# Second MLP of an attention and two-MLP kernel: second products one product later, second high part behind p1, right sums on VectorE, left sums behind a low part

## The reference

```
def _moe2_ref(x, w_a, w_b, w_out):      # x: 2304 x 512, w_a, w_b: 512 x 1536, w_out: 1536 x 512
    a = x @ w_a
    b = x @ w_b
    return (a * b @ w_out).astype(np.float32)
```

## Time and profile before

| what | value |
|---|---|
| median of 3 runs | 998.17 us (997.8 to 999.19) |
| the profiled execution | 996.64 us, span 994.9 us |
| TensorE matmul, weight load | 962.3 us (97%), 899.5 us (90%) |
| VectorE, ScalarE, GpSimd | 609.9, 469.0, 195.4 us |
| lines 704 and 720 (matmuls of the second MLP) | 294.4 and 181.4 us |
| mean granted clock of TensorE | 0.989 of full speed |

### The profile page before, as it was taken

One profiled execution on the slowest core, in us unless ns is written; L12 is line 12 of the kernel. 1 busy time (PEld: TensorE's weight loads), 2 busy tenths in 40 slices (PEclk: granted clock), 3 DMA queues, 4 the chain that ended last, 5 costly groups with the idle time before them and its releaser, 6 DMA issues.

```text
span 994.9 us, 18268 instructions
## 1 busy us (share of the span) xinstructions
PE 962.3 (97%) x6896; PEld 899.5 (90%) x6896; DVE 609.9 (61%) x1075; ACT 469.0 (47%) x1112; POOL 195.4 (20%) x228
## 2 busy tenths in 40 slices
PE   6699999999999999999999999999999999999998
PEld 5589999999999999999999989999889998899996
DVE  5778656556656656555637676556765557656552
ACT  4667544545454545454434544344533334543432
POOL 2200211001210011200034072222262222222210
PEclk9699999999999999999999999999999999999999
DMA  8245220111300122101041132222442222322201
GB/s 197 86 142 148 67 68 19 43 48 38 91 20 22 41 73 61 44 18 50 8 152 33 56 127 64 64 72 70 131 133 74 65 64 64 127 65 64 66 30 64
DMA packets 129351, 71.40 MB, mean 72 GB/s; under 512 B 63248, under 2 KB 120304, under 8 KB 129264
## 3 DMA queue, kind: packets, MB, share of 16 engines
q1 hardware_dynamic: 128224, 69.94, 24.5%
q10 hardware_dynamic: 1040, 0.29, 0.1%
HBM read 60.76 MB, written 9.44 MB: 71 GB/s over the span
## 4 chain that ended last, share of the span: by engine, by line
PE 81%; ACT 8%; DVE 6%; issue 3%; DMA 1%; SPq 0%; POOL 0%; ACTq 0%; DVEq 0%
PE bank L704 23%; PE bank L662 18%; PE bank L648 18%; PE bank L720 14%; ACT sml L763 2%; PE bank L561 2%; PE bank L616 1%; PE bank L567 1%; PE bank L599 1%; PE bank L609 1%; ACT smp L754 1%; DVE wx L1119 1%; PE bank L541 1%; DMA out<-y 1%; DVE wx L1028 1%
## 5 line engine op out<-in xcount | busy, mean ns | idle before, releaser
L704 PE MATMUL bank<-wx 128*128 128x384 f32 x1512 | 294.4, 337 | 1.9 <-DVE c L1112 0.8
L704 PEld LDWEIGHTS bank<-wx 128*128 128x128 f32 x1512 | 268.7, 188 | 19.8 <-ACT u L931 1.6
L648 PE MATMUL bank<-wx 128*128 128x288 f32 x1536 | 231.4, 300 | 0.8 <-ACT relu L851 0.8
L662 PE MATMUL bank<-g_hi,wx 128*128 128x288 f32 x1024 | 231.9, 302 | 0.0
L648 PEld LDWEIGHTS bank<-wx 128*128 128x128 f32 x1536 | 212.3, 190 | 4.6 <-ACT relu L851 1.0
L720 PE MATMUL bank<-wx 128*128 128x512 f32 x648 | 181.4, 398 | 3.7 <-DVE wx L1119 3.1
L662 PEld LDWEIGHTS bank<-g_hi,wx 128*128 128x128 f32 x1024 | 171.4, 188 | 3.5
L1163 POOL TENSOR_TENSOR raw<-raw 128x256 f32<-128x256 f32 x144 | 111.6, 796 | 312.8 <-DMA raw<-in_moe_w_out 309.9
L662 PE MATMUL bank<-g_lo,wx 128*128 128x288 f32 x512 | 151.5, 296 | 0.0
L720 PEld LDWEIGHTS bank<-wx 128*128 128x128 f32 x648 | 116.9, 187 | 23.9 <-DVE wx L1119 10.3
L1033 DVE TENSOR_TENSOR wx<-raw,wx 128x768 fp32r<-128x768 f32 x108 | 106.7, 1014 | 40.3 <-ACT wx L833 39.6
(11 more groups left out here) (69 smaller groups left out, 923.7 us busy)
## 6 DMA issues: line engine op xcount, KB each, us to landing
raw<-in_moe_w_b SPq DMA_DIRECT2D x72, 128.0 KB, 2.2
raw<-in_moe_w_a SPq DMA_DIRECT2D x72, 128.0 KB, 2.3
raw<-in_moe_w_out SPq DMA_DIRECT2D x36, 256.0 KB, 2.8
vnat<-in_v SPq DMA_DIRECT2D x32, 144.0 KB
o_transposed<-o_sb SPq DMA_DIRECT2D x8, 576.0 KB, 3.1
o_raw<-o_transposed SPq DMA_DIRECT2D x6, 768.0 KB, 5.3
out<-y SPq DMA_DIRECT2D x18, 256.0 KB, 2.2
natq<-in_q SPq DMA_DIRECT2D x63, 72.0 KB, 2.1
```

The costliest lines, as they stand in the source:

```text
L648: mm = nc.tensor.matmul(HB[:, 0:HALF], wi(w, kd, f), xs(x, c % 2)[:, kd], start=(kd == 0 and j == 0), stop=(kd == KD - 1 and j == 2))
L662: mm = nc.tensor.matmul(ACC[o][:, 0:HALF], wo(w, f, o), g[:, slot % GB, :], start=(f == 0 and j == 0), stop=(f == F1 - 1 and j == 2))
L704: mm = nc.tensor.matmul(dst, left(w, n, a, kd), right(x, i)[:, kd * HC:(kd + 1) * HC], start=(opens and kd == 0 and m == 0), stop=(kd == K ...
```

## The change

Five edits, which belong together:

- TensorE: the second products of the step before begin behind product 1 instead of product 0; tiles 2 and 3 stand together behind product 3.
- ScalarE: the high part of `prod[1]` of a step stands behind the p1 copy of the next step, instead of behind the high part of `prod[0]`.
- VectorE: c12 stands ahead of the low part of `prod[0]` (but in the last step), and that of `prod[1]` is still last, which now waits for ScalarE's later high part.
- The right operands' sums are VectorE's: one in each of the slots 5 to 8 of the first MLP's last chunk, and one in each of steps 4 to 7 of chunks 0 and 1, ahead of c22.
- GpSimd: from block 3 on, the left sums of block n wait for the low part of `prod[0]` of step n - 3.

```diff
--- before.py
+++ after.py
@@ -728,7 +728,7 @@
                 for i in range(N7):
                     product(n, i)
                     if n > 0:
-                        for tt in ((0,), (1,), (2,), (3,), (4, 5), (), ())[i]:
+                        for tt in ((), (0,), (1,), (2, 3), (4, 5), (), ())[i]:
                             down_2(n - 1, tt)
             for tt in range(TT):
                 down_2(STEPS - 1, tt)
@@ -894,6 +894,12 @@
                 past(act, y_stored[tt % 3], 16 * (2 * c + tt // 3))
                 nc.scalar.activation(y[:, tt % 3, :], ACC2[tt], ACT.Copy).then_inc(y_ready, 1)
 
+            def split_product_hi(n, h):
+                act.wait_ge((pr1_ready, pr2_ready)[h], n + 1)
+                if n >= 2:
+                    p_free(n - 2)
+                nc.scalar.activation(p_hi[:, n % 2, h], prod[h], ACT.Copy).then_inc(ph_ready, 1)
             for n in range(STEPS):
                 c, f = divmod(n, F2)
                 renew = f == F2 - 1 and c + 1 < NC2
@@ -901,6 +907,8 @@
                 act.wait_ge(up_done, N7 * n + 1)
                 past(act, c11_ready, n)
                 nc.scalar.activation(p1_sb, X_BANK, ACT.Copy).then_inc(p1_taken, 1)
+                if n > 0:
+                    split_product_hi(n - 1, 1)
                 if renew:
                     split_right_hi(c + 1, 0)
                 if over:
@@ -931,14 +939,11 @@
                 nc.scalar.activation(u3_sb, X_BANK, ACT.Copy).then_inc(u3_taken, 1)
                 if over:
                     take_y(c - 1, 3)
-                for h, ready in enumerate((pr1_ready, pr2_ready)):
-                    act.wait_ge(ready, n + 1)
-                    if n >= 2:
-                        p_free(n - 2)
-                    nc.scalar.activation(p_hi[:, n % 2, h], prod[h], ACT.Copy).then_inc(ph_ready, 1)
+                split_product_hi(n, 0)
                 if over:
                     take_y(c - 1, 4)
                     take_y(c - 1, 5)
+            split_product_hi(STEPS - 1, 1)
             for tt in range(TT):
                 take_y(NC2 - 1, tt)
 
@@ -1032,6 +1037,13 @@
                 dve.wait_ge(w2_hi, PIECES * n + i + 1)
                 nc.vector.tensor_tensor(piece2(LO, n, i), raw[:, n % RB, LEFT + i * PIECE:LEFT + (i + 1) * PIECE],
                                         piece2(HI, n, i).bitcast(f32), ALU.subtract).then_inc(w2_lo, 1)
+            def right_sum(c, k):
+                name, a, b_ = (("t1", "b12", "b11"), ("t3", "b22", "b12"), ("t2", "b22", "t1"), ("t4", "b21", "t2"))[k]
+                dve.wait_ge(oraw_in, 32 * (c + 1))
+                if k >= 2:
+                    dve.wait_ge(t_ready, 4 * c + 2 * k - 3)
+                nc.vector.tensor_tensor(right_raw(name), right_raw(a), right_raw(b_), ALU.subtract).then_inc(t_ready, 1)
 
             def split_right_lo(c, j):
                 dve.wait_ge(x2h, N7 * c + j + 1)
@@ -1079,11 +1091,18 @@
                 attention(2 * slot + 1)
                 split_g_lo(slot)
                 if c == NCH - 1:
+                    if 5 <= f < 9:
+                        right_sum(0, f - 5)
                     for piece in early_pieces(f):
                         split_w2_lo(*divmod(piece, PIECES))
                     for j in early_rights(f):
                         split_right_lo(0, j)
             take_acc(NCH - 1)
+            def split_product_lo(n, h):
+                dve.wait_ge(ph_ready, 2 * n + 1 + h)
+                nc.vector.tensor_tensor(p_lo[:, n % 2, h], prod[h], p_hi[:, n % 2, h].bitcast(f32), ALU.subtract)\
+                  .then_inc(pl_ready, 1)
 
             for n in range(STEPS):
                 c, f = divmod(n, F2)
@@ -1108,6 +1127,8 @@
                 if n + 2 < STEPS:
                     split_w2_lo(n + 2, 0)
                     split_w2_lo(n + 2, 1)
+                if 4 <= f < 8 and c + 1 < NC2:
+                    right_sum(c + 1, f - 4)
                 dve.wait_ge(u3_taken, n + 1)
                 nc.vector.tensor_tensor(c22_sb, Y_BANK, u3_sb, ALU.add).then_inc(c22_ready, 1)
                 if renew:
@@ -1115,18 +1136,18 @@
                 dve.wait_ge(up_done, N7 * n + 6)
                 dve.wait_ge(c11_ready, n + 1)
                 nc.vector.tensor_tensor(prod[0], X_BANK, c11_sb, ALU.mult).then_inc(pr1_ready, 1)
-                dve.wait_ge(ph_ready, 2 * n + 1)
-                nc.vector.tensor_tensor(p_lo[:, n % 2, 0], prod[0], p_hi[:, n % 2, 0].bitcast(f32), ALU.subtract)\
-                  .then_inc(pl_ready, 1)
+                if n == STEPS - 1:
+                    split_product_lo(n, 0)
                 dve.wait_ge(up_done, N7 * n + 7)
                 dve.wait_ge(u2_taken, n + 1)
                 nc.vector.tensor_tensor(c12_sb, Y_BANK, u2_sb, ALU.add).then_inc(c12_ready, 1)
+                if n < STEPS - 1:
+                    split_product_lo(n, 0)
                 dve.wait_ge(c12_ready, n + 1)
                 dve.wait_ge(c22_ready, n + 1)
                 nc.vector.tensor_tensor(prod[1], c12_sb, c22_sb, ALU.mult).then_inc(pr2_ready, 1)
-                dve.wait_ge(ph_ready, 2 * n + 2)
-                nc.vector.tensor_tensor(p_lo[:, n % 2, 1], prod[1], p_hi[:, n % 2, 1].bitcast(f32), ALU.subtract)\
-                  .then_inc(pl_ready, 1)
+                split_product_lo(n, 1)
 
         @block.gpsimd
         def _(pool):
@@ -1171,28 +1192,16 @@
                 pool.wait_ge(s_ready, 4 * n + 3)
                 sum_of("s4", "a12", "s2", ALU.subtract)
 
-            def right_sums(c):
-                def sum_of(name, a, b_):
-                    nc.gpsimd.tensor_tensor(right_raw(name), right_raw(a), right_raw(b_), ALU.subtract).then_inc(t_ready, 1)
-                pool.wait_ge(oraw_in, 32 * (c + 1))
-                sum_of("t1", "b12", "b11")
-                sum_of("t3", "b22", "b12")
-                pool.wait_ge(t_ready, 4 * c + 1)
-                sum_of("t2", "b22", "t1")
-                pool.wait_ge(t_ready, 4 * c + 3)
-                sum_of("t4", "b21", "t2")
             for slot in range(SLOTS):
                 attention(2 * slot)
                 attention(2 * slot + 1)
             left_sums(0)
             left_sums(1)
-            right_sums(0)
             for n in range(2, STEPS):
+                if n >= 3:
+                    pool.wait_ge(pl_ready, 2 * (n - 3) + 1)
                 left_sums(n)
-                if n % F2 == 4 and n // F2 + 1 < NC2:
-                    right_sums(n // F2 + 1)
 
 
 # ---- launch: one core; inputs and outputs as the reference has them ----
```

## The result

The changed kernel takes 985.24 us (median of 4 runs, 983.96 to 987.05) against 998.03 us: ratio 0.9865, 95% interval 0.9846 to 0.9884. A second measurement of both gave 986.65 us against 998.56 us, 0.9875 (0.9849 to 0.9901). So it is 1.2 to 1.4% faster. The forecast was 987.4 us with a range from 985.6 to 993.5: faster, as forecast.

The account below looks back on a forecast made before the run. TensorE, busy 97% of the span, bounds the kernel, and only 11.2 us of waits could be won; 10.6 us off the 998.17 us median makes 987.6, stated as 987.4 us, range 985.6 to 993.5.

Parts of the forecast that it names:

- The sum: Over the 34 steps: 11.2 us of waits less 0.3 us at each of two chunk starts, 10.6 us gained.
- The chunks' starts: Two steps where ScalarE waits for y's store, 1.45 and 1.31 us over; 0.3 us left at each.
- the bare step: Time TensorE needs between like groups of second products when nothing holds it: 11.53 us.
- the low end of the range: 985.6 us: all 11.2 us of waits gone and 0.02 us per step for the shape, with the scatter of runs.
- Part 1: TensorE's second products one product later, c12 first on VectorE: removes 6.1 us and half 0's low-part delays in four dear steps.
- T: The moment product 0 of a step starts on TensorE; other times in the hand-over are counted from it.
- Rival 2: VectorE between products 6 and 1: c12 late for product 1, 3.5 us per 0.1 us beyond the slack; chance 0.06.
- Rival 3: Nothing changes: another limit of the hand-over stops the later second products too, 997 to 998 us; chance 0.05.
- Part 2 and 3: Second high part behind p1, left sums held back: half 1's low part loses 0.57 us, c11 still in time, priced nothing.
- Rival 1: The collision moves to c11: product 3 waits 0.2 us per step, 6.6 us back, 994 us; chance 0.12.
- Part 4: Right sums on VectorE: 1.05 and 1.26 us come back in two steps; first MLP nothing, up to 0.5 us if misread.

Follow-up runs that it names:

- y_next: Changed kernel with the y copies of tiles 3 to 5 moved one step later, behind the second high part of the chunk's second step; 984.98 us, ratio 0.9856.
- lo_first: Changed kernel with VectorE's old order alone, the low part of half 0 ahead of c12; 1002.61 us, ratio 1.0047.
- hold_only: Kernel before with only the hold of the left sums added; 991.11 us, ratio 0.9916.
- left_free: Changed kernel without the hold on the left sums; 984.62 us, ratio 0.9868.
- hi_first: Changed kernel with ScalarE's old order, both high parts together ahead of the p1 copy; 988.76 us, ratio 0.9897.
- two_orders: Kernel before with two of the five edits, TensorE's new order and c12 ahead of the low part of half 0; 998.14 us, ratio 0.9994.
- right_pool: Changed kernel with the right operands' sums on GpSimd again, behind the left sums of steps 4 and 16; 987.85 us, ratio 0.9884.
- before_again: Kernel before profiled and timed once more, nothing edited; 999.48 us, ratio 1.0006.
- three_orders: Changed kernel without its two GpSimd edits: right sums on GpSimd again, left sums not held; 986.79 us, ratio 0.9873.
- pe_old: Changed kernel with TensorE's old order alone, second products again beginning behind product 0; 998.99 us, ratio 1.0000.

## Why the prediction was right in its steps and wrong in its range

- **The sum.** It said 11.2 us of waits in the steps, 0.6 of them left, 10.6 gained. Measured between the two profiles: 403.26 - 392.73 = 10.53. Two terms were off and cancelled. The chunks' starts kept 1.5 us, not 0.6 (the copy of tile 3 waits for a store that SyncE issues behind the raw loads, and only the two later copies had been thought to matter); y_next, with 0.35 us, shows that 1.1 of them came from there. And the bare step is 11.507 us instead of 11.533, 0.9 us in 34. The quiet steps of every kernel with TensorE's new order take 11.51 or 11.50 (lo_first has none), those of hold_only, with the old one, 11.533; that one change of shape less is the reason, as the forecast and the low end of the range had it, is argued and not shown.
- **Part 1** (second products later, c12 ahead): c12 ended at T + 0.77, 0.75 was said, and it was priced at nothing, rightly; its slack was 0.23 us and not 0.1. Rival 2 did not come. Its price, 3.5 us for each 0.1, was too low: lo_first, 0.35 us beyond the slack, would be 12.3 by it and lost 16.6, for want of the 0.11 us behind every gap.
- **Rival 3** fell: with the second products later, 30 steps take 11.51 us.
- **Part 2 and 3**: the low part of half 1 was said to lose 0.57 us beside a left sum, and loses 1.124 - 0.558 = 0.57; c11 was said to end at T + 4.0, and ends at T + 3.9. (Product 3 starts behind three groups of six and two of three; "four groups" is a slip, the sum has three.) Rival 1 did not come. What the prediction did not see is that these two edits are a cover for each other. With the second high part behind p1 the hold is worth nothing (left_free); with the hold, the high part may stay where it was but for the chunks' starts (hi_first); without both, 402.87 - 394.93 - 2.3 (the right sums) = 5.6 us of waits return, most of them at product 2 (two_orders).
- **Part 4**: right for the steps, by right_pool (2.3 us). For the first MLP the prediction had only asked what the sums would cost VectorE, and found nothing, which is right. That they cost TensorE 1.0 us where they stood, in five of the six profiles with them, it could not see in the earlier trace rows, which come from the sixth: "TensorE had no gap".
- **The step that failed** is the last one of the sum, the way from one profiled execution to the median: "the median of the runs shown lies 1.5 higher, at 998.17, which makes 987.6". The prize of 11.2 us was read from one execution, and what the others take over it was treated as a constant that the change leaves alone. The runs showed three parts in it. The waits: 11.2 us in that execution, 406.57 - 392.1 = 14.5 in before_again. The 1.0 us in the first MLP: absent in that execution, there in before_again. Both go with the change, whatever their size, and should not have been added back. And the beginning, whose other variation (560 to 564 us in executions of either kernel) the change does leave alone, so that the range's low end, built on a beginning of 562.2, should have reached some 2 us lower.
- **How much luck.** Profile against profile, 994.9 - 982.2 = 12.7 us are 10.5 in the steps and 2.1 in the beginning (562.21 - 560.09), and these 2.1 are no effect of the change. The median over all eight executions of the changed kernel in both measurements is 986.0 us, inside the range; that the first four lay at 985.24 is in part luck.

How the 12 to 13 us between the medians divide can be estimated. The beginnings of the fourteen profiles have a mean of 561.9 us without the 1.0 us in the first MLP, and the rest is 31.2. For the kernel before at 998.6 us (the median of two of the measurements) this leaves 998.6 - 31.2 - 562.9 = 404.5 us for the 34 steps, so 12.4 of waits where the forecast had 11.2. That is an estimate; two profiles of the kernel before are too few to measure it.

## What to carry to other kernels

When a wait comes from a chance meeting of two engines, take the distance between like events in the quiet step as the floor and price the change as "all of it goes", for the profiled execution and for the others alike; add back of the difference between profile and median only what the change leaves alone. Look at each moved instruction with the two that stand behind it: here two edits alone brought nothing (two_orders), a third made them worth 1.3% (three_orders), and one reordered line turns the gain into a loss (lo_first). Profile the kernel before more than once if its waits are of this kind. If an engine disturbs a tight hand-over, keeping it away (hold_only) and making room for it (three_orders) are two ways to quiet ordinary steps, and doing both adds nothing there.

## What the runs showed of the hardware

- A VectorE instruction with two SBUF inputs that starts in the middle of a GpSimd sum lasts until that sum's end plus 0.42 us, and the next GpSimd sum then waits in turn: in the changed kernel the low part of half 1 takes 1.12 us in 29 of the 36 steps, and four left sums 4.12 us instead of the 2.94 to 3.14 that most take in the kernel before. prod[1] is held in the same way (1.09 us in two_orders), while c12 and c11, with one input in PSUM, keep 0.54 to 0.56 in every profile.
- A gap on TensorE between these matmuls costs its length and 0.10 to 0.12 us more, since the matmul behind the first one starts late too (179 gaps, pe_old above).
- The moments at which the granted clock falls to 1.2 GHz in the first 60 us differ between executions of the same kernel (mean 0.83 and 0.69 in the two of the kernel before), and so does the time at which the second MLP begins, by up to 4 us (560 to 564). That the one causes the other is not shown. The 4 us are 0.4% of this kernel, about as much as the confidence intervals above are wide.
